# Attention sums computed as channels by tokens, and the experts' weight conversions spread over a tile

## The reference, cut to what matters

```python
def phi(x):                                   # 64 channels -> 256 features
    proj = np.einsum('bhsd,df->bhsf', x, w_phi)            # w_phi 64 x 128
    proj = proj - np.max(np.abs(proj), axis=-1, keepdims=True)
    return np.concatenate([np.exp(proj), np.exp(-proj)], axis=-1)
q_p, k_p = phi(q), phi(k)
kv = np.einsum('bhsf,bhsd->bhfd', k_p, v)                  # 256 x 64 a head
z = np.sum(k_p, axis=2)
num = np.einsum('bhsf,bhfd->bhsd', q_p, kv)
den = np.einsum('bhsf,bhf->bhs', q_p, z)[..., None] + 1e-06
x = num / den                                 # then heads side by side: 4 x 576 x 512
gate = sigmoid(conv over 5 earlier tokens of x)            # channel by channel
x = (gate * (x @ w_val)) @ w_out                           # 512 x 512 each
# each token goes to one of 8 experts e (argmax of gate logits, or the previous token's)
out = p[e] * (relu(x @ w1[e]) @ w2[e])        # w1 512 x 1024, w2 1024 x 512
```

## Time and profile before

| | |
|---|---|
| median of 3 runs | 537.79 us |
| profiled execution | 537.73 us, span 535.9 us |
| TensorE busy | 512.8 us (96%), granted clock 0.993 of 2.4 GHz |
| VectorE, ScalarE, GpSimd busy | 302.3 (56%), 262.4 (49%), 221.6 us (41%) |
| attention, 16 steps | 0 to 159 us |
| value stage, then logits and output stage | 159 to 211 us, then to 269 us |
| expert stage | 272 to 536 us |

### The profile page before, as it was taken

How to read it: one execution, slowest core, us unless ns; L and a number is a source line. 1 busy time by engine, 2 the same in 40 slices (tenths; PEclk the granted TensorE clock), 3 DMA queues, 4 the chain that set the end, 5 groups by cost and what they waited for, 6 DMA issues and landing times.

```text
span 535.9 us, 13321 instructions
## 1 busy us (share of the span) xinstructions
PE 512.8 (96%) x5374; PEld 433.0 (81%) x5374; DVE 302.3 (56%) x492; ACT 262.4 (49%) x450; POOL 221.6 (41%) x224
## 2 busy tenths in 40 slices
PE   6999999999999999999998998999999998999993
PEld 5898999989999997678886676888877786888872
DVE  4686878788986554485516557322465568422221
ACT  2565566766785331544526565222545656422320
POOL 3079999999999931435720011010010102000001
PEclk9999999999999999999999999999999999999998
DMA  8466474745500000008489497111462896111101
GB/s 287 139 209 200 137 242 136 229 156 170 194 4 1 1 1 0 1 1 276 128 289 345 151 349 293 40 39 49 139 244 77 319 321 213 40 39 39 47 32 43
DMA packets 31351, 75.34 MB, mean 141 GB/s; under 512 B 4159, under 2 KB 4415, under 8 KB 31296
## 3 DMA queue, kind: packets, MB, share of 16 engines
q1 hardware_dynamic: 25600, 60.37, 33.6%
q0 software_dynamic: 3104, 9.46, 4.6%
q10 hardware_dynamic: 2592, 4.74, 3.1%
HBM read 57.46 MB, written 17.55 MB: 140 GB/s over the span
## 4 chain that ended last, share of the span: by engine, by line
PE 79%; DMA 8%; DVE 6%; issue 4%; ACT 1%; POOL 1%; POOLq 0%; SPq 0%; ACTq 0%; DVEq 0%
PE turn L662 7%; PE kv_ps L710 7%; DMA sorted_rows<-ytok,pos_i 6%; PE turn L663 6%; PE turn L664 6%; PE pair_ps L671 6%; PE num_ps L662 6%; PE num_ps L729 6%; PE num_ps L664 6%; PE num_ps L663 6%; PE pair_ps L662 3%; PE pair_ps L664 3%; PE pair_ps L663 3%; PE pair_ps L878 3%; PE turn L637 3%
## 5 line engine op out<-in xcount | busy, mean ns | idle before, releaser
L568 POOL TENSOR_TENSOR gate<-gate,tap 128x576 f32<-128x576 f32 x64 | 93.4, 1459 | 5.3
L612 POOL DMA_INDIRECT out_rows<-o_sb,meta_cur x18 | 18.7, 1040 | 153.3 <-DVE o_sb L1444 153.3
L1431 DVE TENSOR_TENSOR h_t<-pair_ps,h_t 128x512 fp32r<-128x512 f32 x36 | 24.9, 691 | 94.3 <-ACT h_t L1174 94.3
L662 PE MATMUL turn<-wts,h_t 128*128 128x512 f32 x144 | 60.8, 422 | 5.0 <-issue 4.3
L662 PE MATMUL num_ps<-wts,y_t 128*128 128x512 f32 x144 | 59.5, 413 | 0.1
L663 PE MATMUL turn<-wts,h_t 128*128 128x512 f32 x144 | 57.6, 400 | 0.0
L664 PE MATMUL turn<-wts,h_t 128*128 128x512 f32 x144 | 57.3, 398 | 0.0
L664 PE MATMUL num_ps<-wts,y_t 128*128 128x512 f32 x144 | 56.9, 395 | 0.0
L663 PE MATMUL num_ps<-wts,y_t 128*128 128x512 f32 x144 | 56.9, 395 | 0.0
L1208 DVE TENSOR_REDUCE absmax<-pair_ps 128x8 f32<-128x1024 f32 x31 | 38.0, 1225 | 30.5 <-PE pair_ps L671 30.5
L1166 ACT ACTIVATE h_sb<-num_ps 128x512 f32<-128x512 f32 x36 | 21.6, 599 | 67.4 <-PE num_ps L664 67.4
(11 more groups left out here) (210 smaller groups left out, 1120.7 us busy)
## 6 DMA issues: line engine op xcount, KB each, us to landing
ring<-in_w SPq DMA_DIRECT2D x36, 512.0 KB, 8.2
stage<-in_w SPq DMA_DIRECT2D x28, 512.0 KB, 5.5
kq_t<-in_kq SPq DMA_DIRECT2D x15, 576.0 KB, 6.3
sorted_rows<-padrow SPq DMA_DIRECT2D x9, 771.0 KB, 5.7
v_sb<-in_v_aug SPq DMA_DIRECT2D x16, 325.0 KB, 3.3
ysl<-sorted_rows ACTq DMA_DIRECT2D x18, 257.0 KB
wout_t<-in_w_out_t SPq DMA_DIRECT2D x1, 1024.0 KB, 9.0
wval_sb<-in_w_val SPq DMA_DIRECT2D x1, 1024.0 KB, 10.3
```

The costliest lines, as they stand in the source:

```text
L568: nc.gpsimd.tensor_tensor(g, g, tap[:, t % 2, :], ALU.add).then_inc(conv_step, 1)
L662: nc.tensor.matmul(dst, x[0], w[0], start=first, stop=False)
```

## The change

The denominators' and numerators' products swap their sides. `kvz` now holds, per feature half and head, 64 columns of z repeated (DEN) and 64 columns of kv (NUM), both stationary; `q_phi` moves, 512 tokens of a head at a time, and 64 for the mixed slab. The results are channels by tokens, the layout of `x_t`; the denominator stands in all 64 channel rows. So the transposes of x, `xo`, and ScalarE's copies into `x_t` go. ScalarE copies `kvz` in two instructions, and copies the denominators with 1e-6 added to `den_sb` (`read_den`, 128 x 512 and 128 x 64). VectorE takes the reciprocal of `den_sb`, 128 x 576 (`invert`), multiplies the 64 mixed columns first, the 512 others after `shift(1)`. The mixed slab's sums lie in `kv_ps` (columns 384 to 511), so that `sum_kv(n, 0)` waits for `edge_ok`, given by the multiplication of the mixed columns of pair n-1. `project_q` moves between the two halves of `sum_kv`, the two exponentials of k are split, `turn_mixed` moves ahead of `sum_kv` and into `mix_ps`. The convolution waits for `normed` instead of ScalarE's copy. `SENT` becomes 6. In the expert stage the eight chunks of a first tile are dealt out as 1, 1, 3 and 3 on both engines, and in the very first tile `turn_y(1)` stands between `down(5)` and `down(6)`, `turn_few` behind `down(7)`.

```diff
-    TURNS = 4
+    TURNS = 3
...
-    xo = place("xo", [P, (FULL + 1) * P], F32, spot["v_sb"])
-    kvz = place("kvz", [P, 2, 2, KVW], F32, spot["xo"])
+    den_sb = place("den_sb", [P, S], F32, spot["v_sb"])
+    kvz = place("kvz", [P, 2, 2, 2, D], F32, spot["den_sb"])
...
-        SENT = 3
+        SENT = 6
...
+        DEN, NUM = 0, 1
+        EDGE = 384
+        def edge(kind):
+            return slice(EDGE + kind * D, EDGE + (kind + 1) * D)
...
-                for i in chunks[6:]:
+                for i in chunks[5:]:
                     split(i)
...
-                pool.wait_ge(turn_read, x_turned(n))
+                pool.wait_ge(normed, n + 1)
...
-            def turn_x(n, number, bank):
...
-            def turn_mixed(n, first):
...
+            def turn_mixed(n, left):
+                pe.wait_ge(shifted_ok, n.times(PROJ, PROJ + 1 if left >= 1 else PROJ))
+                nc.tensor.transpose(mix_ps[:, 2 * FEAT:2 * FEAT + P], shifted[:, SLABS + mixed_at(n), :],
+                                    ident[:]).then_inc(turned, 1)
...
                 if f == 0:
                     pe.wait_ge(v_in[n.k % 2], n.half_count(16))
+                    if not (isinstance(n.loop, int) and n.k == 0):
+                        pe.wait_ge(edge_ok, n.times(1))
...
-            def numerators(n, first):
...
+            def sums(n, kind, part):
+                for f in range(2):
+                    for h in range(2):
+                        rows = slice(h * HALF, (h + 1) * HALF)
+                        if part == 0:
+                            dst = num_ps[rows, kind, :]
+                            src = q_phi[:, f, h * FULL:(h + 1) * FULL, :].rearrange("p s x -> p (s x)")
+                        else:
+                            dst = kv_ps[rows, edge(kind)]
+                            src = q_phi[:, f, MIX, rows]
+                        ins = nc.tensor.matmul(dst, kvz[:, f, h, kind, :], src, start=(f == 0), stop=(f == 1))
+                return ins
+            def all_sums(n, first):
+                pe.wait_ge(kvz_ok, n.times(2, 1))
                 pe.wait_ge(turn_read, number_of(n, 1) + 1)
                 if not first:
                     pe.wait_ge(normed, n.times(1))
...
+                sums(n, DEN, 0)
+                pe.wait_ge(turn_read, number_of(n, 2) + 1)
+                pe.wait_ge(kvz_ok, n.times(2, 2))
+                sums(n, DEN, 1)
+                sums(n, NUM, 1).then_inc(num_ok, 1)
+                sums(n, NUM, 0).then_inc(num_ok, 1)
             def step(n, left):
...
                 for j in range(2):
                     turn_q(n, j)
-                for f in range(2):
-                    sum_kv(n, f)
+                turn_mixed(n, left)
+                sum_kv(n, 0)
+                if left >= 1:
+                    project_q(n + 1)
+                sum_kv(n, 1)
                 if first:
                     make_wog()
-                if left >= 1:
-                    project_q(n + 1)
-                if not first:
-                    turn_x(n + (-1), number_of(n, 2), turn_ps[0])
-                turn_mixed(n, first)
                 if left >= 2:
                     project_mixed(n + 2)
...
-                numerators(n, first)
+                all_sums(n, first)
...
-                    if b == 0 and i == 1:
-                        turn_x(Step(0, PAIRS - 1), ALL_TURNS - 2, turn_ps[0])
...
-                if not early:
-                    turn_y(t + 1)
-                    turn_few()
                 pe.wait_ge(ht_ok, t * 2 + 2)
                 for kk in range(4, KT):
                     ins = down(kk)
+                    if not early and kk == KT - 3:
+                        turn_y(t + 1)
                 ins.then_inc(o_ok, 1)
+                if not early:
+                    turn_few()
...
+                src = kv_ps[:, 0:4 * KVW].rearrange("p (f h x) -> p f h x", f=2, h=2)
+                nc.scalar.copy(kvz[:, :, :, DEN, :], src[:, :, :, D:KVW].to_broadcast([P, 2, 2, D])).then_inc(kvz_ok, 1)
+                nc.scalar.copy(kvz[:, :, :, NUM, :], src[:, :, :, 0:D]).then_inc(kvz_ok, 1)
+            def read_den(n):
+                act.wait_ge(num_ok, n.times(2, 1))
+                nc.scalar.activation(den_sb[:, 0:FULL * P], num_ps[:, DEN, :], ACT.Copy, bias=1e-6).then_inc(den_ok, 1)
+                nc.scalar.activation(den_sb[:, FULL * P:S], kv_ps[:, edge(DEN)], ACT.Copy, bias=1e-6).then_inc(den_ok, 1)
+            def exp_k(n, f):
                 act.wait_ge(shifted_ok, n.times(PROJ, 2))
+                if not (isinstance(n.loop, int) and n.k == 0):
+                    act.wait_ge(kv_summed if f == 1 else kv_half, n.times(1))
...
-                for i in [] if begins else chunks[0:2]:
+                for i in [] if begins else chunks[0:1]:
                     round_weights(i)
...
-                        for i in chunks[2:3]:
+                        for i in chunks[1:2]:
...
-                for i in chunks[3:6]:
+                for i in chunks[2:5]:
                     round_weights(i)
...
+            def invert(n):
+                dve.wait_ge(den_ok, n.times(2, 2))
+                nc.vector.reciprocal(den_sb[:], den_sb[:]).then_inc(inverse_ok, 1)
+                dve.wait_ge(inverse_ok, n.times(1, 1))
+                dve.wait_ge(num_ok, n.times(2, 2))
+                nc.vector.tensor_tensor(x_into(n, FULL * P, HALF), kv_ps[:, edge(NUM)], den_sb[:, FULL * P:S],
+                                        ALU.mult).then_inc(edge_ok, 1)
             def normalise(n):
...
+                nc.vector.tensor_tensor(x_into(n, 0, FULL * P), num_ps[:, NUM, :], den_sb[:, 0:FULL * P],
+                                        ALU.mult).then_inc(normed, 1)
             def step(n, left):
+                later = not (isinstance(n.loop, int) and n.k == 0)
+                if later:
+                    invert(n + (-1))
                 if left >= 1:
                     shift(1, n + 1)
-                if not (isinstance(n.loop, int) and n.k == 0):
+                if later:
                     normalise(n + (-1))
...
-                for i in [] if begins else chunks[0:3]:
+                for i in [] if begins else chunks[0:1]:
                     rest_of_weights(i)
                 for half in range(2):
+                    if half == 1 and not begins:
+                        for i in chunks[1:2]:
+                            rest_of_weights(i)
...
-                for i in chunks[0:1] if begins else chunks[3:6]:
+                for i in [] if begins else chunks[2:5]:
                     rest_of_weights(i)
```

More of the change, by code:

```diff
@@ L245, in attention_moe_kernel @@
         den_ok = sem("den_ok")
+        edge_ok = sem("edge_ok")
+        inverse_ok = sem("inverse_ok")
         normed = sem("normed")
@@ L621, in _ @@
         def _(pe):
[L622 to L629, removed]
             def turn_q(n, j):
@@ L1014, in read_kv @@
                 act.wait_ge(kv_summed, n.times(1, 1))
[L1015 to L1030, removed]
-            def exp_k(n):
+                src = kv_ps[:, 0:4 * KVW].rearrange("p (f h x) -> p f h x", f=2, h=2)
+                nc.scalar.copy(kvz[:, :, :, DEN, :], src[:, :, :, D:KVW].to_broadcast([P, 2, 2, D])).then_inc(kvz_ok, 1)
@@ L1040, in step @@
                 first = isinstance(n.loop, int) and n.k == 0
-                for j in range(2):
+                for j in range(3):
                     act.wait_ge(turned, number_of(n, j) + 1)
                     exp_q(n, j).then_inc(turn_read, 1)
+                if not last:
+                    exp_k(n + 1, 0)
                 read_kv(n)
@@ L1047, in step @@
                     nc.scalar.copy(wogt[:], num_ps[:, 0, 0:P]).then_inc(wog_ok, 1)
-                if not first:
-                    act.wait_ge(turned, number_of(n, 2) + 1)
-                    read_x(n + (-1)).then_inc(turn_read, 1)
-                act.wait_ge(turned, number_of(n, 3) + 1)
-                ins = exp_q(n, 2)
-                if not first:
-                    ins = read_x_mixed(n + (-1))
-                ins.then_inc(turn_read, 1)
-                if first:
                     act.wait_ge(wog_made, 2)
                     nc.scalar.copy(wog[:].rearrange("p c e -> p (c e)"), num_ps[:, 1, 0:P]).then_inc(wog_ok, 1)
+                read_den(n)
                 if not last:
-                    exp_k(n + 1)
-            exp_k(Step(0, 0))
+                    exp_k(n + 1, 1)
+            for f in range(2):
+                exp_k(Step(0, 0), f)
             step(Step(0, 0))
@@ L1215, in shift @@
                 if j == 2 and not (start and n.k == 0):
[L1216 removed]
+                    dve.wait_ge(turned, n.times(TURNS, 2 - TURNS))
                 nc.vector.tensor_tensor(shifted[:, at, :], src, absmax[:, at].unsqueeze(2).to_broadcast([P, w, FEAT]),
                                         ALU.subtract).then_inc(shifted_ok, 1)
[L1220 to L1237 removed]
@@ L1276, in _ @@
```

(3 more changed lines are left out.)

91 lines of the change are left out of this document (21 added, 70 removed).

## The result

The changed kernel takes 592.74 us (median of 4 runs, 585.91 to 594.19) against 537.76 us before: a ratio of 1.101, 95% interval 1.095 to 1.108. It is slower. The forecast was 584 with a range of 553 to 602.

The account below looks back on a forecast made before the run. The prediction took TensorE to bound the kernel before, and a loop through VectorE's reciprocal to set the changed attention step; 537.7 + 51.0 (attention) + 0.5 (value stage) - 5.2 (expert stage) = 584 us, range 553 to 602.

Parts of the forecast that it names:

- The loop from one multiplication of mixed columns to the next: Attention: through shift(1), project_q, sums, copies and the reciprocal, 12.56 us a step, with TensorE's 10.3 us inside it.
- both waits that were named: Attention: TensorE waits ahead of sum_kv(n, 0) and project_q, about 2.2 us of idle time a step in two pieces.
- the cheap: Rival, attention: the reciprocal takes 0.76 us, the step is 10.3 + 0.35, total 555 us; chance 0.13.
- the dear reciprocal: Rival, attention: the reciprocal takes 4.6 us, the loop 13.8, total 602 us; chance 0.09.
- the long rows at full rate: Rival, attention: wide float32 sums cost 0.23 us a two, not 0.43, reciprocal 1.06 ns a value; 531 us; chance 0.04.
- the clock in every step: Rival, attention: idle time lowers the granted clock each step, adding 15 x 1.7 us, total 609 us; chance 0.08.
- The reciprocal: Attention, VectorE: 576 values a partition at 5.6 ns each from the trace's slope, 3.37 us.
- my upper bound: Attention, reciprocal: all that 9 values cost over the ordinary 156 ns goes by value, 7.8 ns each, 4.6 us.
- Value stage: Start of the value stage: TensorE waits about 1 us for VectorE's gating, the last x's transposes leave; plus 0.5 us.
- Expert stage: Expert stage: fewer conversions ahead of down(0) give 3.5 us, the first tile and scatters 1.7; minus 5.2, bounds 0 and 6.0.
- the two DMA waits of the first tile: Expert stage, first tile: waits of 0.9 + 0.8 us, covered by down products and six scatters in flight, gaining 1.7 us.
- Its size in attention: Attention as a whole: it ends at 210.4 us against 159.4, plus 51.0 us.

Follow-up runs that it names:

- the last experiment: The changed kernel with the reciprocal cut into 64, 128 and 384 columns, placed apart on VectorE, same results: 563.97 us, ratio 1.051.
- the filled run: The changed kernel with matmuls that nothing reads, four ahead of sum_kv(n, 0) and four ahead of project_q, in steps 1 to 15: 587.26 us, ratio 1.092.
- The conversions alone: The kernel before with only the chunks dealt out as 1, 1, 3, 3, the first tile's transposes and SENT as before: 531.94 us, ratio 0.992.
- the expert part: The kernel before with chunks as 1, 1, 3, 3, turn_y and turn_few later in the first tile, and SENT = 6: 532.29 us, ratio 0.990.

## Why the prediction was right, point by point

**Direction and mechanism: right.** The loop from one multiplication of mixed columns to the next sets the step, with TensorE idle at both waits that were named. Without the reciprocal the step is 10.8, with its place changed 11.3, with TensorE filled up unchanged. The rivals fall: the cheap and the dear reciprocal by its row, the long rows at full rate by L717 (eight wide records in 1.72 us, 110.25 to 111.97 in the run without the reciprocal, 0.43 us a two, as at L813), the clock in every step by the runs.

**The reciprocal: mis-sized.** It takes 3.753 us, every time, where I had 3.37. From 18 to 576 values the slope is (3753 - 266) / 558 = 6.25 ns a value; my 5.6 came from two short rows, whose difference of 50 ns was too small a base. 0.38 us in fifteen steps is 5.7 us of the 8.7 us between forecast and median. The parts of the last experiment, 64, 128 and 384 values in 0.55, 0.94 and 2.54 us, give 6.1 to 6.3 ns. The estimate made with the Trainium skill's page "VectorE: DVE Perf Modes" (eight clocks, 4.8 us) was further off on the other side; measured is a cost by value that lies between the two. (The slope of my upper bound is 7.7 ns, not 7.8; its 4.6 us stand.)

**The rest of the loop.** The sum was 12.56, the step is 12.79 or 12.59. With the true reciprocal the sum would be 12.94: ScalarE's copies and what lies around them take 0.77 us (128.71 to 129.48) and not 0.90, the multiplication of the mixed columns with its wait 0.28 and not 0.40, and the sums 0.08 more than I had (126.28 to 128.71, 2.43 and not 2.35). That these errors nearly cancel is luck. The steps of 12.79 are those written as a loop, 1 to 8; in the steps written out behind them a dependent VectorE instruction follows within 0.03 us, where I had 0.12 and the loop has 0.12 to 0.15, which makes the 0.2.

**The clock: left at nothing, worth 0 to 8 us.** I put it into a rival with a fall in every step and into the range. The four runs took 592.19, 594.19, 585.91 and 593.29 us at mean clocks of 0.985, 0.982, 0.997 and 0.983. The profiled one has four falls, three of them seen as steps of 14.57, 14.35 and 14.17 us in place of 12.79 and 12.59, 1.6 to 1.8 us each. It is the main part of what separates the median from the forecast beside the reciprocal, and the whole spread. The page "TensorE: Matmul & The Clock Gate" of the Trainium skill (Part 1) says that activity releases the throttle; the filled run agrees, with 587.3 against 592.7 us.

**Value stage.** Plus 0.5 us forecast; 51.8 us from its first matmul to its last against 51.4. TensorE waits 0.72 us for VectorE's first gating behind the last reciprocal.

**Expert stage: right in sum, wrong in its parts.** 5.2 us forecast, 5.7 measured alone. The conversions alone give as much, within noise. The agreement is partly luck: TensorE's waits from 272 us on fall from 7.0 us, the three of the earlier trace rows and two smaller ones,

```profile
PE turn L662 <- DVE h_t L1431: 0.6, 1, 0.6
PE pair_ps L878 <- issue: 0.4, 1, 0.4
```

to 3.9, so by 3.1 us and not 5.2; the rest of the 5.7 seems to be falls of the clock, which the sum left out here (last section). The step of the prediction that failed is that the two DMA waits of the first tile would simply be covered: what came next in that place, ScalarE's five casts ahead of the next tile's relu, was late by the same amount. I had asked it of the changed `down` order and not of the queue of the engine that feeds the next tile.

**Its size in attention.** 51.0 forecast, 54.8 in the filled run (214.1 less 159.3), which has no falls and about 1 us of fillers, 60.0 with four. Of the 2.8 us that are left between them, the longer steps (12.79 and 12.59 for 12.56) make about 2; the rest was not taken apart.

## What to carry to other kernels

A layout that saves transposes can still cost TensorE more than it saves, when a sum that was one column of 65 becomes 64 equal rows: count columns before instructions. An operation whose cost goes by the free size (the reciprocal, 6.25 ns a value) must not stand whole ahead of work that feeds the busiest engine; cut it and place the pieces beside that engine's work, which gave 29 us here with no arithmetic saved, some 23 by the shorter step and the rest by falls of the clock that did not come. When a wait is covered in one queue, look at what each other engine has queued ahead of the next thing needed.

## What the runs showed of the hardware that was not expected

The reciprocal's time does not vary: 3.752 to 3.755 us in sixteen executions. A kernel with more TensorE work had the lower median (587.3 against 592.7 us), because about 2 us of idle time a step in two pieces was enough for the granted clock to fall now and then, and its falls alone made a spread of 8 us in four runs. They also lie in the kernel before: the two of its runs beside the experiments with a mean clock of 0.996 and 0.997 took 534.69 and 533.55 us, the others, at 0.989 to 0.994, 535.6 to 539.1. The runs with the expert part or the conversions alone have 0.994 to 0.997. So about half of the expert stage's 5 to 6 us is idle time that is gone, and the other half, by these runs, falls of the clock that such idle times had brought on the earlier trace rows; this split was read from the runs and not tried by itself.
